# Seven identity products before the queries, two value pieces exchanged between VectorE and POOL, pooling steps re-dated, and the last step's joins reordered

## The reference

```python
# 1: attention over pooled keys and values; q, k, v are 8 x 8 x 576 x 64
k_p = k.reshape(B, H, 72, 8, D).mean(axis=3)      # each 8 rows of k and of v averaged
v_p = v.reshape(B, H, 72, 8, D).mean(axis=3)
scores = matmul(q, k_p.T) / sqrt(D)
attn = softmax(scores)                             # minus max, exp, over (sum + 1e-9)
x = matmul(attn, v_p)                              # then reshaped to 4608 x 512
# 2: soft mixture of experts, 8 experts of 4 slots, phi 512 x 32
logits = x @ phi
slot_input = softmax_over_tokens(logits).T @ x
slot_out[e] = relu(slot_input[e] @ w1[e]) @ w2[e]
x = softmax_over_slots(logits) @ slot_out          # 4608 x 512
# 3: squared-ReLU MLP
h = x @ w_in                                       # 512 -> 2048
out = (s * relu(h)**2 + b) @ w_out                 # 2048 -> 512
```

## Time and profile before

| | us |
|---|---|
| median of 3 runs | 664.7 (663.92 to 665.53) |
| profiled execution, its own time | 658.32 |
| its span, first to last instruction | 656.4 |
| TensorE busy | 629.1 (96%) |
| VectorE busy | 479.2 (73%) |
| ScalarE busy | 449.5 (68%) |
| POOL busy | 126.1 (19%) |
| mean granted TensorE clock | 0.987 |

### The profile page before, as it was taken

How to read it: one execution, slowest core, us unless ns; L and a number is a source line. 1 busy time by engine, 2 the same in 40 slices (tenths; PEclk the granted TensorE clock), 3 DMA queues, 4 the chain that set the end, 5 groups by cost and what they waited for, 6 DMA issues and landing times.

```text
span 656.4 us, 16681 instructions
## 1 busy us (share of the span) xinstructions
PE 629.1 (96%) x6466; PEld 546.1 (83%) x6466; DVE 479.2 (73%) x791; ACT 449.5 (68%) x753; POOL 126.1 (19%) x127
## 2 busy tenths in 40 slices
PE   7788999999999999989999999999999999999995
PEld 7566777777753338879999999999999999999995
DVE  5756676566445639876888888888888887888876
ACT  1577777777522259986777777777777777777771
POOL 3899687732210020002100000000000000000000
PEclk9799999999999999999999999999999999999998
DMA  9787959584379970000100000000000000000001
GB/s 335 246 247 290 382 184 421 149 351 171 130 271 408 414 318 1 1 0 17 50 32 18 33 16 32 16 32 16 32 16 29 19 32 16 16 32 26 23 18 64
DMA packets 26004, 80.49 MB, mean 123 GB/s; under 512 B 6496, under 2 KB 14688, under 8 KB 23392
## 3 DMA queue, kind: packets, MB, share of 16 engines
q1 hardware_dynamic: 25952, 79.76, 32.7%
HBM read 70.32 MB, written 9.44 MB: 122 GB/s over the span
## 4 chain that ended last, share of the span: by engine, by line
PE 86%; DVE 4%; DMA 3%; POOL 2%; ACT 2%; issue 2%; DVEq 0%; ACTq 0%; POOLq 0%
PE bank L1846 16%; PE bank L1836 16%; PE bank L1835 16%; PE bank L1752 5%; PE bank L1610 4%; PE bank L1775 2%; PE bank L1534 2%; PE bank L1778 2%; PE bank L1695 2%; PE bank L1597 2%; PE bank L1716 2%; PE bank L1782 2%; PE bank L1567 2%; DMA kvbuf<-in_k_dram 2%; PE bank L1640 2%
## 5 line engine op out<-in xcount | busy, mean ns | idle before, releaser
L1318 DVE TENSOR_TENSOR lo_sb<-a_sb,hi_sb 128x896 fp32r<-128x896 f32 x128 | 140.1, 1094 | 56.3 <-PE bank L1846 55.1
L1004 ACT ACTIVATE hi_sb<-a_sb 128x896 fp32r<-128x896 f32 x128 | 122.2, 955 | 78.6 <-PE bank L1836 74.0
L1835 PE MATMUL bank<-w_hi,hi_sb 128*128 128x256 f32 x384 | 97.7, 283 | 0.0
L1836 PE MATMUL bank<-w_lo,hi_sb 128*128 128x256 f32 x384 | 97.7, 283 | 0.0
L989 ACT ACTIVATE a_sb<-r_sb 128x512 f32<-128x512 f32 x144 | 91.1, 632 | 6.4
L1846 PE MATMUL bank<-w_hi,lo_sb 128*128 128x256 f32 x384 | 87.8, 283 | 0.0
L982 ACT ACTIVATE r_sb<-bank 128x512 f32<-128x512 f32 x144 | 83.5, 580 | 0.0
L1835 PEld LDWEIGHTS bank<-w_hi,hi_sb 128*128 128x128 f32 x384 | 73.7, 192 | 0.0
L1836 PEld LDWEIGHTS bank<-w_lo,hi_sb 128*128 128x128 f32 x384 | 73.7, 192 | 0.0
L1846 PEld LDWEIGHTS bank<-w_hi,lo_sb 128*128 128x128 f32 x384 | 64.5, 192 | 0.0
L1836 PE MATMUL bank<-t_early,hi_sb 128*128 128x256 f32 x256 | 64.2, 283 | 0.0
(11 more groups left out here) (187 smaller groups left out, 1273.8 us busy)
## 6 DMA issues: line engine op xcount, KB each, us to landing
early_third<-in_moe_w_dram SPq DMA_DIRECT2D x5, 2048.0 KB, 12.2
kvbuf<-in_k_dram SPq DMA_DIRECT2D x12, 768.0 KB, 5.4
kvbuf<-in_v_dram SPq DMA_DIRECT2D x12, 768.0 KB, 6.5
out_dram<-o_sb SPq DMA_DIRECT2D x36, 256.0 KB, 2.3
qbuf<-in_q_dram SPq DMA_DIRECT2D x8, 1024.0 KB, 8.6
early<-in_moe_w_dram SPq DMA_DIRECT2D x4, 2048.0 KB, 12.1
late<-in_moe_w_dram SPq DMA_DIRECT2D x3, 2048.0 KB, 14.2
after_last<-in_moe_w_dram SPq DMA_DIRECT2D x2, 2048.0 KB, 9.2
```

The source lines that it names most:

```text
L1004: act.activation(hi_sb[:, n % 2, :], a_sb[:, n % ARING, P:2 * CH], ACT.Copy).then_inc(hi_ready, 1)
L1318: dve.tensor_tensor(lo_sb[:, n % 2, :], a_sb[:, n % ARING, P:2 * CH], hi_sb[:, n % 2, :].bitcast(F32), ALU.subtract).then_inc(lo_ready, 1)
L1835: pe.matmul(acc, hi, rhs_hi, start=(k == 0 and (at == AT1 or at % 2 == 1)), stop=False, skip_group_check=True)
L1836: last = pe.matmul(acc, hi, rhs_lo, start=False, stop=False, skip_group_check=True)
```

## The change

1. TensorE: 7 identity products instead of 9, after keys (0,0) and before the loop, not at the end of step 0.
2. Value piece (0,0) goes to POOL and (0,1) to VectorE, in its step 1, its copy now a reduction over a dimension of one. Value piece (1,0) goes from POOL to VectorE: three groups in steps 5, 6 and 7 and a copy in step 7.
3. Pooling steps of pairs 1 and 2 are re-dated. POOL, pair 1: from 3,4,4,5,5,6,6,7,7,8 to 3,4,4,5,6,7,7,8; pair 2: from 8 to 17, one part each, to 10,11,12,12,13,14,15,16,17,17; pair 3 stays (17 to 26). VectorE's keys of pair 2: from steps 8, 9, 10 to 10, 11, 11.
4. SP: `load_q(1, 0)` stands before the value loads of pair 1.
5. Last step of the last group: TensorE finishes each block in turn (hi-hi, hi-lo, lo-hi), after the low parts are ready. `last_joins` takes the place of the joins; POOL adds the row to the two halves of the right tile's addend and to the left half of the left tile; SP stores the right tile first.

```diff
-    START_WARM = 9
+    START_WARM = 7
@@ dve_keys, pool_parts
-                steps = (3, 4, 4) if i == 1 else tuple(TPP * i - 10 + g for g in range(GP))
+                steps = ((3, 4, 4), (10, 11, 11), tuple(TPP * PAIRS - 19 + g for g in range(GP)))[i - 1]
+        def dve_values(n):
+            return [g for g in range(GP) if 5 + g == n]
-                steps = (3, 4, 4, 5, 5, 6, 6, 7, 7, 8) if i == 1 else tuple(TPP * i - 10 + x for x in range(10))
-                pieces = ((0, 1), (0, 2), (1, 0), (1, 1), (1, 2))
+                pieces = [(which, u) for which, u in ((0, 1), (0, 2), (1, 0), (1, 1), (1, 2)) if not (which and values_by_dve(i, u))]
+                steps = ((3, 4, 4, 5, 6, 7, 7, 8), (10, 11, 12, 12, 13, 14, 15, 16, 17, 17),
+                         tuple(TPP * PAIRS - 19 + x for x in range(10)))[i - 1]
         def values_by_dve(i, u):
-            return i == 0 and u == 0
+            return (i, u) in ((0, 1), (1, 0))
@@ SP
+            load_q(1, 0)
             for u in range(PIECES):
                 load_kv(1, 1, u)
-            load_q(1, 0)
...
+            sp.wait_ge(last_joined, JOINS)
+            store(HALVES - 1, 1)
+            sp.wait_ge(last_left_ready, 1)
+            sp.wait_ge(out_ready, 2 * HALVES - 1)
+            store(HALVES - 1, 0)
@@ POOL
-            for which, u in ((0, 1), (1, 1), (1, 2)):
+            for which, u in ((0, 1), (1, 0), (1, 2)):
                 halve(which, 0, u)
                 pool_rest(which, 0, u)
...
+            pool.wait_ge(last_joined, 1)
+            pool.tensor_tensor(pu_sb[:, 0, :], pu_sb[:, 0, :], row_b[:, left], ALU.add).then_inc(last_row_added, 1)
+            pool.wait_ge(last_joined, 3)
+            pool.tensor_tensor(pu_sb[:, 1, :], pu_sb[:, 1, :], row_b[:, right], ALU.add).then_inc(last_row_added, 1)
+            pool.wait_ge(last_joined, 4)
+            pool.tensor_tensor(last_tile[:, left], last_tile[:, left], row_b[:, left], ALU.add).then_inc(last_left_ready, 1)
@@ VectorE
-                dve.tensor_copy(groups[:, :, 1, :], groups[:, :, 0, :]).then_inc(v_pooled_dve, 1)
+                dve.reduce_sum(groups[:, :, 1, :], groups[:, :, 0, :].unsqueeze(3), AX.X).then_inc(v_pooled_dve, 1)
+            def pool_values_group(g):
+                slot, loads = kv_piece(1, 1, 0)
+                dve.wait_ge(kv_in[slot], 16 * loads)
+                dve.wait_ge(vT_ready, PIECES)
+                dve.reduce_sum(vp[:, g, 0, :], kv_groups(slot, g), AX.X).then_inc(v_pooled_dve, 1)
+                if g == GP - 1:
+                    dve.wait_ge(v_pooled_dve, GP + 2)
+                    dve.tensor_copy(vp[:, 0:GP, 1, :], vp[:, 0:GP, 0, :]).then_inc(v_pooled_dve, 1)
-            pool_values(0)
@@ end of VectorE's step n
+                if n == 1:
+                    pool_values(1)
                 for i, u, g in dve_keys(n):
                     pool_keys(i, u, g)
+                for g in dve_values(n):
+                    pool_values_group(g)
@@ last_joins (its waits on the blocks, in order)
+                dve.wait_ge(half_ready, c * PARTS7 + AT7 + 1)
+                scaled_sum(x_sb[:, :], half_bank(1, AT6), s_col, pu_sb[:, 0, :]).then_inc(last_joined, 1)
...
+                scaled_sum(u3_sb[:, :], half_bank(1, AT7), minus_s, x_sb[:, :]).then_inc(last_joined, 1)
+                dve.wait_ge(half_ready, c * PARTS7 + AT5 + 1)
+                scaled_sum(pu_sb[:, 1, :], half_bank(1, AT5), s_col, x_sb[:, :]).then_inc(last_joined, 1)
...
+                scaled_sum(tile(0), found_of(AT4), s_col, u3_sb[:, :].unsqueeze(1).to_broadcast([P, 2, LEFT])).then_inc(last_joined, 1)
+                dve.wait_ge(half_ready, c * PARTS7 + PARTS7)
+                dve.wait_ge(last_row_added, 2)
...
+                scaled_sum(tile(1), found_of(AT2), s_col, pu_sb[:, :, :]).then_inc(last_joined, 1)
+                dve.wait_ge(last_joined, 4)
+                o = o_sb[:, tiles[0], LEFT:D]
+                dve.tensor_tensor(o, o, row_b[:, LEFT:D], ALU.add).then_inc(out_ready, 1)
@@ TensorE
             turn_keys(0, 0, 0)
+            for _ in range(START_WARM):
+                pe.matmul(bank[A_B[0]][:, 0:P], ident[:, :], ident[:, :], start=True, stop=True)
...
-                    for _ in range(START_WARM):
-                        pe.matmul(bank[A_B[0]][:, 0:P], ident[:, :], ident[:, :], start=True, stop=True)
...
+            def last_step_products(n, k):
+                pe.wait_ge(lo_ready, step(HALVES - 1, k) + 1)
+                for at, lhs, rhs_hi, rhs_lo in half_blocks(k):
+                    hi, lo = (parts7[:, n % 2, P * lhs:P * (lhs + 1)] for parts7 in (hi_sb, lo_sb))
+                    pe.matmul(half_bank(1, at), hi, rhs_hi, start=False, stop=False, skip_group_check=True)
+                    pe.matmul(half_bank(1, at), hi, rhs_lo, start=False, stop=False, skip_group_check=True)
+                    pe.matmul(half_bank(1, at), lo, rhs_hi, start=False, stop=True, skip_group_check=True).then_inc(half_ready, 1)
```

More of the change, by code:

```diff
@@ L362, in pooled_attention_soft_moe_squared_relu_kernel @@
         row_done = sem("row_done")
+        last_joined = sem("last_joined")
+        last_row_added = sem("last_row_added")
+        last_left_ready = sem("last_left_ready")
         out_ready = sem("out_ready")
@@ L484, in pool_parts @@
             for i in range(1, PAIRS):
-                steps = (3, 4, 4, 5, 5, 6, 6, 7, 7, 8) if i == 1 else tuple(TPP * i - 10 + x for x in range(10))
-                pieces = ((0, 1), (0, 2), (1, 0), (1, 1), (1, 2))
-                at += [(pieces[x // 2][0], i, pieces[x // 2][1], x % 2) for x in range(10) if steps[x] == n]
+                pieces = [(which, u) for which, u in ((0, 1), (0, 2), (1, 0), (1, 1), (1, 2)) if not (which and values_by_dve(i, u))]
+                steps = ((3, 4, 4, 5, 6, 7, 7, 8), (10, 11, 12, 12, 13, 14, 15, 16, 17, 17),
+                         tuple(TPP * PAIRS - 19 + x for x in range(10)))[i - 1]
+                at += [(pieces[x // 2][0], i, pieces[x // 2][1], x % 2) for x in range(2 * len(pieces)) if steps[x] == n]
             return at
@@ L515, in values_pooled @@
             if values_by_dve(i, u):
-                return v_pooled_dve, 2
-            return v_pooled, 2 * (PIECES * i + u)
+                return v_pooled_dve, (GP + 3 if i else 2)
+            return v_pooled, 2 * (PIECES * i + u - (1 if i else 0)) if i else u + 2
         MISC_USES = sorted([(U + 5, 0, "logits", sum(closes_logits(o) for o in range(U + 1))) for U in range(UNITS) if closes_logits(U)] +
@@ L743, in _, with store @@
                 sp.dma_start(tile_rows(m), o_sb[:, m, :]).then_inc(stored[m], 16)
-            for c in range(HALVES):
+            def store(c, m):
+                sp.dma_start(tile_rows(MT + 2 * c + m), o_sb[:, 2 * (c % 2) + m, :]).then_inc(stored[2 * (c % 2) + m], 16)
+            for c in range(HALVES - 1):
                 for m in range(2):
                     sp.wait_ge(out_ready, 2 * c + m + 1)
-                    sp.dma_start(tile_rows(MT + 2 * c + m), o_sb[:, 2 * (c % 2) + m, :]).then_inc(stored[2 * (c % 2) + m], 16)
+                    store(c, m)
+            sp.wait_ge(last_joined, JOINS)
[3 more added lines that the diff above has]
+            store(HALVES - 1, 0)
             for m in range(MT):
@@ L757, in _ @@
             pool.memset(phi_bd[:, :, :], 0.0).then_inc(phi_zero, 1)
-            PARTS = [(which, 0, u, part) for which, u in ((0, 1), (1, 1), (1, 2)) for part in range(2)]
+            PARTS = [(which, 0, u, part) for which, u in ((0, 1), (1, 0), (1, 2)) for part in range(2)]
             PARTS += [part for n in range(STEPS) for part in pool_parts(n)]
@@ L823, in _ @@
                 pool.tensor_tensor(o_sb[:, m, :], o_sb[:, m, :], row_b, ALU.add).then_inc(out_first, 1)
+            left, right, last_tile = slice(0, LEFT), slice(LEFT, D), o_sb[:, 2, :]
+            pool.wait_ge(last_joined, 1)
[4 more added lines that the diff above has]
+            pool.tensor_tensor(last_tile[:, left], last_tile[:, left], row_b[:, left], ALU.add).then_inc(last_left_ready, 1)
         @block.scalar
@@ L1421, in _ @@
             add_row(HALVES - 2, 0, 1)
-            for n in range(4):
-                join(HALVES - 1, 1, n)
-            add_row(HALVES - 1, 1, 0)
-            join(HALVES - 1, 1, 4)
-            add_row(HALVES - 1, 1, 1)
+            last_joins()
         @block.tensor
@@ L1821, in steps @@
                         pe.wait_ge(t_lo_ready, k + 1)
+                    if final and k == KP - 1:
+                        last_step_products(n, k)
+                        continue
                     if k == 0:
```

14 lines of the change are left out of this document (added).

## The result

| | before | after |
|---|---|---|
| median (executions) | 664.31 us (4) | 654.12 us (4) |
| ratio, 95% interval | | 0.9868 [0.9832, 0.9904] |
| profiled execution, own time | 658.32 | 654.17 |
| its span | 656.4 | 652.2 |

The account below looks back on a forecast made before the run. TensorE, busy 96% of the span, was taken as the bound, so gains lie where it waits: front 3.3 plus end 1.8 is 5.1 us, 664.7 - 5.1 = 659.6. Range 656.9 to 663.1, the forecast's own 658.2 to 661.2.

Parts of the forecast that it names:

- The base, and the range: Whole kernel: gains from the profiled execution subtracted from the runs' median 664.7; range 656.9 to 663.1.
- Units 0 to 6: Attention's start: first scores at 14.4 us, unit 3's at 27.2, 0.8 earlier; unit 4's at 33.0.
- rival 3: Front: half clock comes earlier and stays up to 33 us; gain only 2.5, time 662.2; chance 8%.
- VectorE's steps 6 and 7: VectorE's attention loop: 3.65 us with value group and logits copy, 1.03 for piece (1,0)'s copy; half a us lost by unit 7.
- The front term, 3.3: Attention up to unit 12: its scores start at 65.9 us instead of 69.22, a gain of 3.3.
- Step 11 costs it 5.2 us against TensorE's 4.6: Front, step 11: VectorE's key groups of pair 2 make it slower than TensorE, giving back half a us.
- From unit 12 on each step is as it was: Attention behind the front: step intervals unchanged from unit 12 on, so the front's gain of 3.3 us is kept.
- The end, 1.8: Behind TensorE's last products: last data ready 2.0 us earlier, 0.2 back in the stores; gain 1.8, bounds 0.7 to 2.1.
- Edits costed at nothing: Front: identity products moved into the wait for queries cost nothing; pair 1's queries asked for earlier hold nothing behind them.
- 1 (VectorE bound, value load 2 us later): Steps 5 to 11: VectorE waits 1.9 us more for value piece (1,0), copy 0.8 longer; gain 2.4, 662.3; chance 14%.
- 4 (that load stands in front of the loop): Step 5: VectorE waits for value piece (1,0) without reserve; at the longest landing 2.2 us slower, 666.9; chance 6%.
- 2 (the front at the full clock): Front: TensorE stays at full clock, 2.8 us more gain, less 0.6 eaten by VectorE's loop; 657.4; chance 10%.

Follow-up runs that it names:

- e2: The changed kernel, unedited, timed again beside the kernel before: mean 656.87 us, ratio to before 0.9918.
- e9: The changed kernel, unedited, timed a third time in a later group: mean 657.51 us, ratio to before 0.9923.
- e4: The kernel before with only the new end (part 5 of the change): mean 660.71 us, ratio to before 0.9989.
- e1: The kernel before, unedited, timed again beside itself: mean 663.80 us, ratio to before 1.0026.
- e3: The changed kernel without part 5, so with the old end: mean 657.18 us, ratio to before 0.9929.
- e6: The changed kernel with nine identity products at the end of step 0 again: mean 657.87 us, ratio to before 0.9919.
- e11: The changed kernel with the queries of pair 1 loaded behind that pair's value loads again: mean 656.74 us, ratio to before 0.9927.
- e7: The changed kernel with value piece (0,0) back on VectorE and (0,1) on POOL: mean 658.03 us, ratio to before 0.9929.
- e8: The changed kernel with value piece (1,0) back on POOL, in steps 3 to 8: mean 659.01 us, ratio to before 0.9949.
- e10: The changed kernel with the old pooling dates of pair 2: mean 656.90 us, ratio to before 0.9914.
- e5: The changed kernel with 13 more identity products where TensorE waits for the first two value pieces: mean 659.50 us, ratio to before 0.9944.

## Why the prediction was wrong

**The base, and the range.** This is the step that failed most. "The runs' median is 664.7. I take differences from the first and subtract them from the second", with "0.5 for the runs' spread". Three executions within 1.6 us hid a scatter with a standard deviation of 2.2 to 3.0 us: in long series before has medians of 662.5 to 664.0. Subtracting from a sample at the upper side set the forecast 1 to 2 us high; the four executions of after then were at its lower side (mean 654.7, against 657.2 over the 24 of e2 and e9). Of the 5.5 us of the miss 2.4 lie between the forecast and those 657.2, and 3.1 are the draw of the four executions. With a deviation of 2.5 us the mean of three has an error of 1.4, the mean of four 1.25, their difference 1.9: to hold 8 times in 10 the range had to be 2.4 us wider to each side, and would then have reached down to 654.5, still 0.4 short. The gain itself, forecast as 5.1, was 5.2 and 5.4 by means in the two long series, 5.1 and 5.4 by their ratios; that it came out so well is in part luck, as the terms show.

**Units 0 to 6** came out as worked out: first scores 14.54 (14.4 forecast), unit 3 at 27.11 (27.2), unit 4 at 32.97 (33.0), the wait for piece (1,0) 0.82 ending at 36.85 (0.8, 36.8), maximum of unit 5 at 37.98 (37.9). For units 3 and 4 that is this execution's luck with the clock (rival 3 below). POOL's normalisation 0 came at 23.95, not 22.8, since POOL stood 1.29 us for the load of value piece 2 (row at 19.89), which I had taken as landed; it did not delay unit 3.

**VectorE's steps 6 and 7.** A step with a value group was priced at 3.65; from the maximum of unit 5 to that of 6 it took 3.08, and to that of 7, copy included, 3.63. So the maxima of units 6 and 7 started at 41.06 and 44.69, for 41.5 and 46.2. The copy of piece (1,0) took 0.40, not 1.03. What it costs is what is left of POOL's instruction: in all 17 traces that have such a copy it starts inside one and ends 0.14 to 0.15 us behind it, 1.03 to 1.06 where it meets a halving of 1.81 early, 0.40 where it meets the last 0.25 of a normalisation. That is the exclusion that the prediction reckons with, and its end of 0.35 for the copy was the near one.

**The front term, 3.3.** Mis-sized: 4.1 to 5.6 in five executions. At unit 12 after is 2.3 us ahead of the forecast (63.63, not 65.9): 1.5 of it is there at the maximum of unit 7, as above, the rest comes in units 8 to 12. "Step 11 costs it 5.2 us against TensorE's 4.6" took the intervals of before as TensorE's own, but there VectorE's key groups had set them. Units 8, 9 and 10 took 3.83, 3.99 and 4.06 us in after, 4.75, 4.33 and 4.57 before. No term counted the low stretch at 48 us, which before has and after has not; that it came of VectorE's 4.46 us wait isn't shown (e4 has both, e1 has the wait, 4.37, and no low stretch there).

**"From unit 12 on each step is as it was"** failed: 1.7 us on the mean went again, by code blocks that came late and the half clock behind them. The two errors nearly cancel, by luck: 4.6 less 1.7 is 2.9 for the forecast 3.3.

**The end, 1.8.** 1.6 in the profiled pair: VectorE's 2.0 came as forecast, but 0.4 of it went in the stores, for 0.2 counted. POOL's additions kept 0.73 (0.74, 0.72, 0.72), uncontended as I took them. The Trainium skill (SBUF — State Buffer, Who interferes with whom) has that a VectorE instruction with one input in SBUF doesn't contend with POOL; by that rule the trace agrees. The timed halves (1.6 for e4 against before, 0.3 for e2 against e3) can't confirm the size.

**Edits costed at nothing**, the identity products (e6) and the queries (e11), show no difference in time, to within some 2 us; in its one trace e6 is 3.1 us late at unit 12, through its products at the half clock. The exchange of pieces (e7) and piece (1,0) on VectorE (e8), which had no terms of their own, bring 1.7 to 2.9 at unit 12 in the traces and some 0.3 and 1.3 us in time, within the error.

**Rivals.** 1 (VectorE bound, value load 2 us later) and 4 (that load stands in front of the loop) fell: VectorE waited 0.82 us for it, in e7 0.95, in e10 1.07. 2 (the front at the full clock) is what e5 brings about: unit 12 comes 1.4 us earlier than in after, not 2.2, and the kernel is no faster. 3 (the clock falls earlier, unit 3's 0.8 is gone) didn't occur in after, and in part in the other traces of its front: in e2, e9 and e11 the low stretch began at 17.3 to 19.2 us and lasted 10.2 for after's 6.8, and unit 3 is at 28.05, 27.85 and 27.96, as late as before (28.04, e1 28.13). It ended by 29.5, not at 33, and the rest of the gain was there.

## What to carry to other kernels

Take the scatter from a long series, together with the slope of time against granted clock, before a few per mille are forecast; three runs that agree are no measure of it. A step's interval in a trace belongs to the engine that ended last in it: when that engine's work is taken out, redo the walk with the next engine's own time. A gain in a front is only as good as what follows: here code blocks arriving late beside a full data queue took a third of it back, and moving the weights moved the loss and, without the fill, made it larger. When an engine stands in the middle of a group and no semaphore ends it, look whether a packet of the instruction queue ends just ahead. Before two traces are compared by stages, take off such stalls and half of the time at the half clock: what is left agreed here within 1 us over 100 where the raw intervals differed by 4.5.

## What the runs showed of the hardware that was not expected

- TensorE stood up to 4.88 us at the border of two code blocks, without any wait in the program; each of 42 stands ended 1.25 to 1.61 us behind the 16 KB packet of the next block. The half clock followed 8 of the 14 stands of 1.0 us or more.
- One identical kernel spreads over 8 to 14 us in 30 to 35 executions; 0.35 to 0.49 us of span for each us at the half clock.
- SP stood 3.6 to 4.5 us in one issue of 768 KB, that of keys (3,0), in all 13 traces with the old place of the weights, and 0.33 in the 5 with a matrix moved away from ahead of it.
- A VectorE copy of 128x192 took 1.03 us in one place and 0.40 in another; in each of 17 traces it ended 0.14 to 0.15 us behind the POOL instruction that it started in.
